# A causal mask written by VectorE's predicated copy in place of TensorE matmuls

## The reference, cut to what matters

```python
for e in range(E):
    q, k, v = x @ wq[e], x @ wk[e], x @ wv[e]
    scores = scale * (q @ k.transpose(0, 2, 1))
    causal = np.triu(np.ones((S, S), dtype=bool), 1)
    scores = np.where(causal, -1000000000.0, scores)
    scores = scores - scores.max(-1, keepdims=True)
    a = np.exp(scores)
    a /= a.sum(-1, keepdims=True) + 1e-09
    ye = a @ v @ wo[e]
    # ... weighted by the gate and summed over the experts
```

## Time and profile before

| | |
|---|---|
| median of 3 runs | 709.44 us (708.34 to 709.71) |
| the profiled execution | 708.54 us, its span 706.8 us |
| TensorE busy | 685.7 us, 4864 matmul instructions |
| VectorE busy | 385.2 us, 753 instructions |
| ScalarE busy | 320.0 us, 805 instructions |
| GpSimd busy | 153.4 us, 199 instructions |
| clock granted to TensorE, mean | 0.993 of full |

### The profile page before, as it was taken

The page is one execution under the profiler, slowest core; times in us unless marked ns, Lnnn a source line. Parts: engine busy times, 40 slices in busy tenths (PEclk is TensorE's granted clock), DMA queues, the critical chain, the costliest instruction groups (busy, mean ns, idle before and its releaser), DMA issues.

```text
span 706.8 us, 12410 instructions
## 1 busy us (share of the span) xinstructions
PE 685.7 (97%) x4864; PEld 448.2 (63%) x4864; DVE 385.2 (55%) x753; ACT 320.0 (45%) x805; POOL 153.4 (22%) x199
## 2 busy tenths in 40 slices
PE   7979999999999999999999999999999999999998
PEld 7866656666656665666656665666665666566554
DVE  7897985282854656537463737636475222551200
ACT  3455546623464246652356424665145614563340
POOL 7672620062201610016010522004420000000000
PEclk9988999999999999999999999999999999999999
DMA  9997500005400080000800034000000000000000
GB/s 235 295 339 194 170 3 1 1 1 137 128 1 1 24 240 1 1 1 24 240 2 1 1 118 146 2 1 1 34 1 2 0 24 12 1 1 11 23 0 35
DMA packets 36922, 43.37 MB, mean 61 GB/s; under 512 B 2560, under 2 KB 27264, under 8 KB 36608
## 3 DMA queue, kind: packets, MB, share of 16 engines
q1 hardware_dynamic: 36864, 42.57, 20.6%
HBM read 37.84 MB, written 4.72 MB: 60 GB/s over the span
## 4 chain that ended last, share of the span: by engine, by line
PE 90%; DVE 3%; DMA 2%; issue 1%; SPq 1%; ACT 1%; POOL 1%; DVEq 0%; ACTq 0%; POOLq 0%
PE bank L923 78%; PE bank L927 6%; PE bank L1086 3%; PE bank L1082 3%; DMA wvg_sb<-in_wvg 2%; DVE idec L651 1%; SPq L246 1%; ACT k_sb L442 1%; ACT shared L460 0%; DVE nmax L679 0%; SPq L258 0%; DVE att L712 0%; POOL rk_sb L345 0%; DVE shared L692 0%; SPq L239 0%
## 5 line engine op out<-in xcount | busy, mean ns | idle before, releaser
L923 PE MATMUL bank<-wv_sb,k_sb 128*128 128x384 f32 x384 | 139.4, 497 | 0.0
L923 PE MATMUL bank<-xk_sb,wk_sb 128*128 128x384 f32 x384 | 138.1, 499 | 0.0
L923 PEld LDWEIGHTS bank<-xk_sb,wk_sb 128*128 128x128 f32 x384 | 68.4, 190 | 42.9 <-issue 5.5
L923 PEld LDWEIGHTS bank<-wv_sb,k_sb 128*128 128x128 f32 x384 | 67.5, 190 | 38.8 <-issue 3.7
L651 DVE RECIPROCAL idec<-dec 112x260 f32<-112x260 f32 x48 | 82.8, 1754 | 0.5
L451 ACT ACTIVATE shared<-bank,nmax 128x128 f32<-128x128 f32 (+5 forms) x96 | 59.9, 628 | 46.9 <-DVE nmax L679 46.9
L679 DVE TENSOR_REDUCE nmax<-bank 128x1 f32<-128x128 f32 (+5 forms) x96 | 55.4, 619 | 46.0 <-PE bank L923 45.9
L376 POOL TENSOR_TENSOR state<-state,carry 112x512 f32<-112x512 f32 x20 | 21.9, 1097 | 264.8 <-DVE state L731 136.2
L923 PE MATMUL bank<-xT_sb,wqk_sb 128*128 128x384 f32 (+1 forms) x240 | 64.1, 424 | 1.1 <-ACT xT_sb L498 0.6
L481 ACT ACTIVATE att<-ident,bonus 128x128 f32<-128x128 f32 x192 | 58.8, 397 | 13.1 <-DVE bonus L659 10.5
L672 DVE TENSOR_TENSOR out_sb<-bank,sg_sb 128x384 f32<-128x384 f32 x24 | 13.4, 557 | 85.2 <-PE bank L923 84.9
(11 more groups left out here) (91 smaller groups left out, 920.9 us busy)
## 6 DMA issues: line engine op xcount, KB each, us to landing
rk_sb<-in_rk SPq DMA_DIRECT2D x24, 384.0 KB, 6.8
v_sb<-in_v SPq DMA_DIRECT2D x24, 256.0 KB, 7.3
w_sb<-in_wT SPq DMA_DIRECT2D x24, 227.5 KB, 5.2
r_sb<-in_rT SPq DMA_DIRECT2D x24, 224.0 KB, 5.0
k_sb<-in_kT SPq DMA_DIRECT2D x24, 224.0 KB, 6.1
out<-out_sb SPq DMA_DIRECT2D x24, 192.0 KB, 1.9
wk_sb<-in_w_k SPq DMA_DIRECT2D x1, 1536.0 KB, 10.7
wv_sb<-in_w_v SPq DMA_DIRECT2D x1, 1536.0 KB, 15.9
```

Source lines behind the costliest of these rows:

```text
L923: return nc.tensor.matmul(out, lhsT, rhs, start=start, stop=stop)
```

## The change

The two bf16 constants `ident_b` and `later_b` go, and with them the mask matmuls. GpSimd fills a new constant `masked_out`, 128 x 128 fp32, with -1e30. The last score matmul of each expert now raises `score_psum`. VectorE waits for both experts, then one `copy_predicated` writes -1e30 over the diagonal blocks of both (2 x 128 elements a partition, in PSUM) where the existing constant `before` is true, raises a new semaphore `score_masked`, waits for it, and takes the two maxima. For blocks 0 to 3 the banks are laid out anew, so that the two experts of a step are neighbours: bank 2 * (i % 2) + e.

```diff
@@ scores / new helper
             if qt_of(h, i) < 4:
-                lo = 2 * e + i % 2
+                lo = 2 * (i % 2) + e
                 return bank[:, lo, :]
             return bank[:, 2 * e:2 * e + 2, :].rearrange("p a x -> p (a x)")
+
+        def diagonal_blocks(h, i):
+
+            lo = qt_of(h, i) * P
+            if h == 0:
+                return bank[:, 2:4, lo:lo + P]
+            if lo < 512:
+                return bank[:, 2 * (i % 2):2 * (i % 2) + 2, lo:lo + P]
+            return bank[:, 1:4:2, lo - 512:lo - 512 + P]
@@ gpsimd
-            g.memset(ident_b[:, :], 0.0)
-            g.memset(later_b[:, :], 0.0)
+            g.memset(masked_out[:, :], NEG)
...
-            for m in (ident, ident_b):
-                g.affine_select(out=m[:, :], in_=m[:, :], compare_op=ALU.not_equal, fill=1.0, base=0,
-                                pattern=[[-1, P]], channel_multiplier=1)
-
-            g.affine_select(out=later_b[:, :], in_=later_b[:, :], compare_op=ALU.is_ge, fill=NEG, base=0,
+            g.affine_select(out=ident[:, :], in_=ident[:, :], compare_op=ALU.not_equal, fill=1.0, base=0,
                             pattern=[[-1, P]], channel_multiplier=1)
@@ vector
             def maxima(h, i):
                 w = width(h, i)
+                dve.wait_ge(score_psum, h * TILES + 2 * i + 2)
+                d.copy_predicated(diagonal_blocks(h, i), bc(before[:, :].bitcast(mybir.dt.int32).unsqueeze(1), [P, 2, P]),
+                                  bc(masked_out[:, :].unsqueeze(1), [P, 2, P])).then_inc(score_masked, 1)
+                dve.wait_ge(score_masked, h * STEPS + i + 1)
                 for e in range(2):
                     n = 2 * i + e
-                    dve.wait_ge(score_psum, h * TILES + n + 1)
                     d.tensor_reduce(nmax[:, n:n + 1], scores(h, i, e)[:, 0:w], axis=AX.X, op=ALU.max, negate=True).then_inc(max_ready, 1)
@@ tensor
-                        mm(scores(h, i, e)[:, lo:hi], qk_sb[rows, m, q0:w], qk_sb[rows, QM + m, lo:hi], stop=hi != w)
-                for e in range(2):
-                    mm(scores(h, i, e)[:, q0:w], ident_b[:, :], later_b[:, :], start=False).then_inc(score_psum, 1)
+                        x = mm(scores(h, i, e)[:, lo:hi], qk_sb[rows, m, q0:w], qk_sb[rows, QM + m, lo:hi])
+                        if hi == w:
+                            x.then_inc(score_psum, 1)
```

More of the change, by code:

```diff
@@ L5 @@
 F32 = mybir.dt.float32
-BF16 = mybir.dt.bfloat16
 ALU = mybir.AluOpType
@@ L127, in build @@
         ident = sb("ident", [P, P])
-        ident_b = sb("ident_b", [P, P], BF16)
-        later_b = sb("later_b", [P, P], BF16)
+        masked_out = sb("masked_out", [P, P])
         before = sb("before", [P, P])
@@ L198, in build @@
         score_psum, max_ready, prob_ready = sem("score_psum"), sem("max_ready"), sem("prob_ready")
+        score_masked = sem("score_masked")
         prob_scaled = sem("prob_scaled")
```

## The result

The changed kernel takes 710.62 us (median of 13 runs, 708.74 to 712.69), the kernel before in the same comparison 708.7 us (13 runs, 708.0 to 709.9). The ratio is 1.0025, with a 95% interval of 1.0017 to 1.0034: +1.8 us, between +1.2 and +2.4. The forecast was +1.7 us (711.1).

A forecast was written before the change was run, and what follows sets the result against it. TensorE, 97% busy, was read as the bound, though most mask pairs stood beside waits for ScalarE. Odd halves 0.7, even halves 0.6 and half 0 0.4 made +1.7 us on the 709.44 median: 711.1 us, range 708.2 to 714.6.

The forecast's parts named there:

- The price of a copy: On VectorE: each of the 48 added predicated copies takes 462 ns, with 419 and 728 ns as ends.
- C + 0.035: Copy of 462 ns plus 0.035 us behind it: first maximum 0.50 us later where VectorE had work.
- Odd halves: h = 1, 3, 5, 7: 0.82 us lost by output(0), 0.645 back in steps 3 to 5; +0.18 each, +0.7 together.
- Even halves: h = 2, 4, 6: later exponentials delay output(0), removing masks frees nothing; +0.20 us each, +0.6 for three.
- Half 0: h = 0: two copies add 1.0 us, the lower clock halves it, mask pairs return 0.1; net +0.4 us.
- the relu's slack at steps 4 and 5: Odd halves, i = 4 and 5: slack used up; copies of 728 ns would cost some 0.27 us more.
- The case of a dear copy: Rival: a VectorE copy with its completion wait is nearer 0.73 us; +5 to +7 us, 714.4 to 716.4; 14%.
- TensorE gets its time back: Rival: VectorE's delay ends in ScalarE's idle time; -2.4 us, 707.0, or 699.1 if all pairs counted; 14% by either.
- point of decision: TensorE gets its time back once exponentials(1) are under 0.2 us late, so a copy under about 0.15.
- The clock's stretch: Rival: a second lower-clock stretch loses 4 us, 715, 8%; without the first, up to 4 won, 706 to 709, 4%.
- no change: Whole kernel: a result within 0.2%, 1.4 us; chance 0.35, against 0.52 for slower and 0.13 for faster.

The follow-up runs named there:

- the fastest: ScalarE's square moved behind its copies, predicated copies only in steps 2 to 5 of halves 1 to 7, mask matmuls elsewhere; 700.76 against 708.84 us before.

## Why the prediction was right

**The price of a copy.** Predicted 462 ns, measured 448 in the mean, 434 in the median, with one of 1234 in it. From the copy's start to the maximum's start it is 0.46 us (441.19 to 441.65), where C + 0.035 gave 0.50 from the point where VectorE would have begun the maximum. The estimate of 392 ns from the Trainium skill (VectorE: DVE Perf Modes, "The TRN2 errata") was too low, as for the longer copy; the row it was worked out from is for a PSUM source, and this copy reads SBUF and writes PSUM. The Trainium skill has it that a semaphore between VectorE instructions costs nothing extra (VectorE: DVE Perf Modes, "The DRAIN you can't avoid"). This trace does not agree: the maximum starts 0.03 behind the copy's end, and chained without a wait 0.08 ahead of it (445.26 and 444.34 + 1.00).

**Odd halves.** Step by step as written: 0.81 lost up to output(0) (predicted 0.82), 3 x 0.215 gained, +0.16 net in halves 3, 5 and 7 (predicted 0.18). The experiments with copies in steps 0 and 1 alone and in steps 3 to 5 alone take the two apart. Half 1 came out at -0.05: its output(0) was already late before, 0.35 behind the end of its scores (106.66 and 106.31) against 0.15 in half 5, so up to there it lost 0.61 and not 0.81. That was in the trace and I counted all four as one. But the 0.20 hangs on half 0 and not on half 1's own copies: with copies in half 0 alone half 1 is 0.20 shorter than before, and with matmuls in half 0 and copies behind it half 1 loses 0.32. What half 0 leaves behind that does this was not followed up.

**Even halves.** Predicted +0.20, measured +0.15 in each. The kernel without any mask shows that the pairs there stood inside a wait for ScalarE, which was the main claim; the square moved aside shows which wait it was.

**Half 0.** This is the term that was mis-sized. Two copies were priced 0.50 each on VectorE; they took 0.46 and 1.27, because GpSimd was at work beside the second, and the transposes came 1.35 later and not 1.0. That the lower clock takes about half of an added microsecond away again was right in kind: with the stretch at the same place 0.8 of the 1.35 is left, where the prediction had 0.4 left of its 1.0, after 0.1 won back. The condition, that the stretch ends when it did, did not hold in the profiled execution of the changed kernel: it began 1.2 later behind score(0), and the half lost 1.44.

**The sum.** That +1.7 met +1.8 so closely is in part luck. Halves 1 to 7 were to lose 1.3 us and lost 0.9 in the profiled execution (2.87 - 1.99), half 0 was to lose 0.4 and lost twice that or more, and 0.42 came back at the end for which there was no term. The errors have both signs and cancel.

**A bound that was wrong.** I wrote that the relu's slack at steps 4 and 5 is used up with nothing left. A second copy took only 0.07 us there. What the step left out: a late relu only matters through the copy behind it, and at those steps output waited for nothing. In half 5 of the kernel before, the copies ended at 457.41 and 463.59, 0.56 ahead of output at 457.97 and 464.15. The case of a dear copy (+5 to +7) was therefore priced too high; by this its lower part was the right one.

**The rivals.** That TensorE gets its time back fell: exponentials(1) are 0.81 late, four times its point of decision, and TensorE alone would have had 2.9 us, not 10.3. The dear copy fell. The clock's stretch moved in time but not in length in the profiled execution. In the timed runs it can be longer: four of the changed kernel's 13 have a mean granted clock of 0.990, below all others, and lie at 710.62 to 712.69. Without them the median is 710.39, so the clock does not make the +1.8. The bound of "no change" was 1.4 us; the measured +1.8 lies outside it, on the side that had the larger chance, though its interval (+1.2 to +2.4) reaches inside.

## What to carry to other kernels

An instruction on the busiest engine is worth only what the instruction behind it gains; ask of each occurrence what that one waited for. Here 30 of the 42 pairs of halves 1 to 7 gave nothing that lasted, and the other 12 gave 0.215 us each. The cost of the replacement is read in the same way, on the other engine's queue: two of the six copies in an odd half made all of its loss. So make such a change by place, and look first for the order on the third engine that holds the result up: with one ScalarE instruction moved and the places chosen, a loss of 1.8 us became a gain of 8.3.

## What the runs showed of the hardware

A VectorE predicated copy with both inputs in SBUF, begun 0.10 us after a GpSimd product of two SBUF tensors (1.05 us), took 1.23 us in place of 0.43 and ended 0.28 us after GpSimd, in all four profiled kernels that have a copy at that place. Two maxima out of PSUM at the same place kept their 0.49 us.

A stretch with TensorE's clock at its lower level (1.2 GHz) comes in half 0 of every profiled execution (two of them in one), and its length is not the same from one to the next. Busy us by engine in it, granted clock third from last, of the changed kernel, of the one without a mask and of the fastest:

```profile
49.50:59.80 10.30, 7.21 (x68) 4.96 (x71) 9.80 (x28) 3.07 (x12) 3.71 (x5) 0.50 1.04 265
```

```profile
45.80:59.50 13.70, 11.55 (x97) 7.74 (x98) 10.68 (x29) 4.50 (x17) 4.66 (x6) 0.50 1.04 281
```

```profile
45.80:52.10 6.30, 2.80 (x22) 2.13 (x24) 6.01 (x16) 1.41 (x7) 3.61 (x5) 1.00 1.13 244
52.10:58.90 6.80, 6.36 (x78) 4.21 (x78) 4.84 (x14) 2.50 (x9) 1.05 (x1) 0.50 1.08 313
```

10.3 us in the first (10.2 before), 13.7 and 6.8 in the others. In the fastest kernel TensorE had been busy 2.80 of the 6.3 us ahead of the fall. Eight profiled executions have the same half 0, with its mask by matmuls; from score(0) of half 0 to that of half 1 they take 55.34 to 56.78 us. So one execution can differ from another by 1.4 us by half 0 alone, nearly as much as the change made. The runs of the changed kernel spread further (708.74 to 712.69), and what else makes that spread is not shown.
